# Query tiles of causal block attention moved by one 64-row block in a fused attention, gating and MLP kernel

## What is computed

```python
scores = (q @ k.T) / 8                       # per batch and head, 576 x 576
mask = (pos // 64)[:, None] >= (pos // 64)[None, :]
attn = softmax(where(mask, scores, -1e9))
x = attn @ v                                 # heads side by side: 4 x 576 x 512
h = relu(x @ w_in); u, v = h[..., :512], h[..., 512:]
v_n = (v - mean(v)) / sqrt(var(v) + 1e-6)
gated = u * (w_spatial @ v_n + b_spatial)
x = gated @ w_out
xn = (x - mean(x)) / sqrt(var(x) + 1e-6) * g_ln
out = x + relu(xn @ w_ch1) @ w_ch2
```

## Time and profile before

| what | value |
| --- | --- |
| median of three timed runs | 792.93 us (792.04 to 794.08) |
| the profiled execution | 791.29 us, of which the span of the trace is 789.5 us |
| PE busy | 778.3 us, 99% of the span |
| DVE, ACT, POOL busy | 63%, 48%, 50% |
| chain that ended last | PE 87%, DVE 6%, ACT 4%, issue 3% |

### The profile page before, as it was taken

The page is one execution under the profiler, slowest core; times in us unless marked ns, Lnnn a source line. Parts: engine busy times, 40 slices in busy tenths (PEclk is TensorE's granted clock), DMA queues, the critical chain, the costliest instruction groups (busy, mean ns, idle before and its releaser), DMA issues.

```text
span 789.5 us, 14255 instructions
## 1 busy us (share of the span) xinstructions
PE 778.3 (99%) x5088; PEld 669.1 (85%) x5088; DVE 497.2 (63%) x1028; ACT 380.5 (48%) x970; POOL 394.4 (50%) x508
## 2 busy tenths in 40 slices
PE   8999999999999999999999999999999999999998
PEld 6767888778887788879988989988898889898987
DVE  7886746366563665528767776688656687545445
ACT  5996675456564565524353333443342345333431
POOL 4886655334353243503356455656454556554541
PEclk9999999999999999999999999999999999999999
DMA  6453332312123220041263231003100000300002
GB/s 233 149 177 95 113 103 77 102 58 72 54 73 102 71 68 25 1 135 53 69 195 112 68 119 54 28 1 120 54 27 1 1 1 33 129 0 1 1 1 81
DMA packets 38149, 56.40 MB, mean 71 GB/s; under 512 B 3136, under 2 KB 20544, under 8 KB 38080
## 3 DMA queue, kind: packets, MB, share of 16 engines
q1 hardware_dynamic: 38080, 55.49, 21.5%
HBM read 46.04 MB, written 9.44 MB: 70 GB/s over the span
## 4 chain that ended last, share of the span: by engine, by line
PE 87%; DVE 6%; ACT 4%; issue 3%; POOL 0%; ACTq 0%; POOLq 0%; DVEq 0%
PE psum L1391 24%; PE psum L1392 23%; PE psum L1393 23%; PE psum L1312 5%; PE psum L1357 4%; ACT probs L808 3%; PE psum L1372 2%; DVE neg_max L1035 2%; PE psum L1377 2%; PE psum L1473 1%; DVE mix_buf L1110 1%; PE psum L1443 1%; PE psum L1426 0%; PE psum L1424 0%; DVE stats L1089 0%
## 5 line engine op out<-in xcount | busy, mean ns | idle before, releaser
L759 POOL TENSOR_TENSOR wp_r<-block,wp_r 128x256 fp32r<-128x256 f32 x168 | 133.7, 803 | 168.3 <-ACT wp_r L941 166.0
L1216 DVE TENSOR_TENSOR sums<-psum,sums 128x384 f32<-128x384 f32 x216 | 113.6, 554 | 105.8 <-PE psum L1393 105.1
L969 ACT ACTIVATE h_r<-sums 128x384 fp32r<-128x384 f32 x96 | 50.4, 526 | 228.8 <-PE psum L1393 119.1
L691 POOL TENSOR_SCALAR probs<-probs,row_inv 128x512 f32<-128x512 f32 (+4 forms) x160 | 92.5, 593 | 108.5 <-DVE row_inv L1048 108.5
L1035 DVE TENSOR_REDUCE neg_max<-psum 128x1 f32<-128x512 f32 (+4 forms) x160 | 80.7, 538 | 58.1 <-PE psum L1312 57.0
L1393 PE MATMUL psum<-w_r,h_r 128*128 128x512 f32 x288 | 114.2, 397 | 0.0
L1392 PE MATMUL psum<-w_r,h_r 128*128 128x512 f32 x288 | 113.7, 395 | 0.0
L1391 PE MATMUL psum<-operand,wp_r 128*128 128x384 f32 x336 | 113.2, 337 | 0.2 <-DVE sums L1216 0.2
L1392 PE MATMUL psum<-operand,wp_r 128*128 128x384 f32 x336 | 113.0, 336 | 0.0
L1393 PE MATMUL psum<-operand,wp_r 128*128 128x384 f32 x336 | 112.4, 334 | 0.0
L808 ACT ACTIVATE probs<-psum,neg_max 128x512 f32<-128x512 f32 (+4 forms) x160 | 89.9, 567 | 45.8 <-DVE neg_max L1035 43.6
(11 more groups left out here) (119 smaller groups left out, 1614.0 us busy)
## 6 DMA issues: line engine op xcount, KB each, us to landing
qk_raw<-qk SPq DMA_DIRECT2D x32, 576.0 KB, 4.0
block<-w_ch SPq DMA_DIRECT2D x32, 256.0 KB, 3.7
y_res<-y_scratch SPq DMA_DIRECT2D x18, 256.0 KB, 3.6
out<-y_res SPq DMA_DIRECT2D x18, 256.0 KB, 2.1
v_raw<-vN SPq DMA_DIRECT2D x16, 256.0 KB, 2.8
y_scratch<-mix_buf SPq DMA_DIRECT2D x16, 256.0 KB, 2.0
y_ring<-y_scratch SPq DMA_DIRECT2D x16, 256.0 KB, 2.7
w_raw<-w_in SPq DMA_DIRECT2D x8, 256.0 KB, 4.3
```

The costliest lines, as they stand in the source:

```text
L691: pool.tensor_scalar(probs[:, n % 2, c], probs[:, n % 2, c], row_inv[:, n % 2, AT[t]:AT[t] + 1], 1.0, ALU.mult, ALU.mult).then_inc(normed, 1)
L759: pool.tensor_tensor(wp_lo[:, n % WP], w1[i % BLOCKS][:, WEIGHT[j]], wp_hi[:, n % WP].bitcast(F32), ALU.subtract).then_inc(wp_lo_done, 1)
L1216: dve.tensor_tensor(dst, product_bank(i, j), other, ALU.add).then_inc(c_summed, 1)
```

## The change

Tiles are moved by 64 rows. Tile 0 is now the first block alone (64 queries, 64 keys, called OWN); tiles 1 to 4 have 128 rows and begin at 64, 192, 320 and 448, with 192, 320, 448 and 576 keys. `score_head` does tiles 1 to 4 in one group of ten matmuls (the keys of tile 4 beyond 512 and those of tile 2 beyond 256 are matmuls of their own, because of banks and quadrants), in banks 0 to 2, with one wait of PE for its own first results in the middle; `score_first` does tile 0's one matmul, into a mixer bank up to head 8 and the output bank later. Counters are now `scored_wide` (tiles 4, 3), `scored_narrow` (1, 2) and `scored_own`.

For t = 1 to 4 only the t full 128 x 128 pieces are transposed per tile; the 64 x 64 blocks on the diagonal of all five tiles are five small transposes, counted as tile OWN. Order of tiles: 4, 3, 1 in step 0, 2 and OWN in step 2, followed by `score_first(n + 1)`. Maxima and exponentials of head n + 1: all four big tiles before the copies in heads 0 to 7; later 4 and 3 before and 1 and 2 after them. OWN's follow in step 2. DVE copies tiles 4 and 2, ACT 3, 1 and OWN. Exponentials of tiles 1 to 4 are plain two-dimensional accesses. `attend` gets a further wait, for all exponentials of the next head. In the mixer heads GpSimd splits weights in step 0 instead of step 1. The empty slot of batches 0 and 2 moves from step 0 of the head after the eight to step 1 of the eighth head; three w groups move by one slot.

```diff
...
-KEYS = [min(P * (t + 1), S) for t in range(NT)]
+KEYS = [BLOCK + P * t for t in range(NT)]
+QUERY_AT = [0] + [BLOCK + P * (t - 1) for t in range(1, NT)]
...
-    pt = place("pt", PT_STEP * NT + P * (NT - 1))
+    pt = place("pt", S * NT)
+    pt_own = pt.rearrange("p (j n) -> p j n", j=NT)[:, :, 0:BLOCK]
...
-    DVE_TILES, ACT_TILES = [3, 1], [0, 2, 4]
+    OWN = 0
+    DVE_TILES, ACT_TILES = [4, 2], [3, 1, OWN]
     def t_place(n, t):
-        if t == NT - 1 and n < H:
-            return m_bank[:, 1, 0:NT * LAST]
-        at = KEYS[2] if t == 0 else 0
-        return t_bank[:, 0 if t in (3, 1) else 1, at:at + (t + 1) * ROWS[t]]
+        if t == 4:
+            return t_bank[:, 0, 0:4 * P]
+        if t == 3:
+            return t_bank[:, 1, 0:3 * P]
+        if t == 1:
+            return t_bank[:, 1, 3 * P:4 * P]
+        late_banks = m_bank if n < H else t_bank
+        return late_banks[0:BLOCK, 1, 0:NT * BLOCK] if t == OWN else late_banks[:, 0, 0:2 * P]
     def transposed_free(pe, n, t):
-        if t == 3 and n >= 1:
-            pe.wait_ge(t_copied_dve, len(DVE_TILES) * n)
-        elif t == 0 and n >= 1:
-            pe.wait_ge(t_copied_act, len(ACT_TILES) * n)
-        elif t == 1:
+        if t == 2 and n >= H:
-        elif t == 4 and n >= H:
+        elif t == OWN and n >= H:
-        elif t == 4 and n >= 1:
-            pe.wait_ge(t_copied_act, len(ACT_TILES) * n)
-    TILES = [3, 0, 2, 1, 4]
-    PEAKS = {3: 1, 0: 3, 2: 3, 1: 5, 4: 5}
+    TILES = [4, 3, 1, 2, 0]
-    MADE = {3: 1, 0: 3, 2: 3, 1: 4, 4: 5}
-    FIRST = 3
-    def second_in_mixer(n):
-        return n <= H
-    def second_banks(n):
-        return psum[:, 2:4, :] if second_in_mixer(n) else psum[:, 1:3, :]
+    FIRST, TURNED = 4, 3
+    WIDE = TILES[:2]
+    PEAKS = {4: 2, 3: 2, 1: 4, 2: 4, 0: 5}
+    def early(n):
+        return FIRST if n < H else len(WIDE)
+    MADE = {4: 1, 3: 3, 1: 3, 2: 4, OWN: 5}
+    SCORES = 5
     def score_of(n, t):
+        flat = psum.rearrange("p a n -> p (a n)")
-            return psum[:, 1, KEYS[2]:KEYS[2] + KEYS[0]]
-        if t == 2:
-            return psum[:, 1, 0:KEYS[2]]
-        if t == 3:
-            return psum[:, 0, 0:KEYS[3]]
-        if t == 1:
-            return second_banks(n)[:, :, pair_at(n):pair_at(n) + P]
-        return second_banks(n)[LAST:P, :, last_at(n):last_at(n) + HALF]
-    def pair_at(n):
-        return S - LAST - P if second_in_mixer(n) else 0
-    def last_at(n):
-        return 0 if second_in_mixer(n) else P
+            return (m_bank[:, 1, :] if n <= H else o_bank)[BLOCK:P, 7 * BLOCK:8 * BLOCK]
+        start = {4: 0, 3: KEYS[4], 2: KEYS[4] + KEYS[3], 1: KEYS[4] + KEYS[3] + KEYS[2]}[t]
+        return flat[:, start:start + KEYS[t]]
     def unseen():
-        for t in (3, 2, 0):
-        for n in (0, HEADS - 1):
+        return [score_of(0, t)[0:BLOCK, KEYS[t] - BLOCK:KEYS[t]] for t in TILES[:NT - 1]]
     def parts(t):
-        return slice(LAST, P) if t == NT - 1 else slice(0, P)
+        return slice(BLOCK, P) if t == 0 else slice(0, P)
+    SPARE = sum(len(r) for r in GROUP_STEPS[:H - 1])
     def groups_at(n, step):
-        return [(at // GROUPS, at % GROUPS)] if at >= 0 and in_batch(at // GROUPS, at % GROUPS) else []
+        b, g = at // GROUPS, at % GROUPS
+        if b % 2 == 0 and g >= SPARE:
+            return [(b, g - 1)] if g > SPARE else []
+        return [(b, g)] if at >= 0 else []
     def late(n, step, lag):
...
         def load_qk(n):
-                sp.wait_ge(scored_second, 4 * (n - QS + 1))
+                sp.wait_ge(scored_wide, SCORES * (n - QS + 1))
+                sp.wait_ge(scored_narrow, SCORES * (n - QS + 1))
+                sp.wait_ge(scored_own, n - QS + 1)
+                    for i in pieces_at(n - 1) if n >= H else []:
+                        split_piece(i)
                 elif step == 1 and n + 1 < HEADS:
-                    for i in pieces_at(n - 1):
+                    for i in pieces_at(n - 1) if n < H else []:
...
-                act.wait_ge(t_made, NT * (n - 2) + AT[t] + 1)
+                act.wait_ge(t_made, NT * (n - 1))
-            dst = probs[r, s, P_AT[t]:P_AT[t] + k]
-            if t in TILES[FIRST:]:
-                dst = dst.rearrange("p (a n) -> p a n", a=2)
-            act.activation(dst, score_of(n, t), ACT.Exp, bias=neg_max[r, s, AT[t]:AT[t] + 1],
+            act.activation(probs[r, s, P_AT[t]:P_AT[t] + k], score_of(n, t), ACT.Exp, bias=neg_max[r, s, AT[t]:AT[t] + 1],
         def copy_transposed(n, t):
-            w = ROWS[t]
-            src = t_place(n, t).rearrange("p (j q) -> p j q", q=w)
-            act.activation(pt_rows(t, t + 1), src, ACT.Copy).then_inc(t_copied_act, 1)
+            act.activation(pt_rows(t), t_blocks(n, t), ACT.Copy).then_inc(t_copied_act, 1)
         def output_right(n):
...
                 if step == 0:
-                        for t in TILES[:FIRST]:
+                        for t in TILES[:early(n)]:
-                    copy_transposed(n, 0)
-                    copy_transposed(n, 2)
+                    copy_transposed(n, 3)
+                    copy_transposed(n, 1)
+                    if n + 1 < HEADS:
+                        for t in TILES[early(n):FIRST]:
+                            exp_tile(n + 1, t)
                 elif step == 1:
                 elif step == 2:
-                    copy_transposed(n, 4)
+                    copy_transposed(n, OWN)
...
                 if step == 0:
-                        for t in TILES[:FIRST]:
+                        for t in TILES[:early(n)]:
-                    invert(n, 1)
+                    if n >= 1:
+                        invert(n, 1)
-                    copy_transposed(n, 3)
+                    copy_transposed(n, 4)
+                    if n + 1 < HEADS:
+                        for t in TILES[early(n):FIRST]:
+                            max_tile(n + 1, t)
                 elif step == 1:
                 elif step == 2:
+                    copy_transposed(n, 2)
-                    copy_transposed(n, 1)
...
-        def seen(n, t, half, upper):
-            query = 2 * t + upper
-            k = BLOCK * (query + 1)
-            return score(n, score_of(n, t)[HIGH if upper else LOW, 0:k], half, query, slice(0, k))
+        def seen(n, t, half, upper, start=0, end=512):
+            query = QUERY_AT[t] // BLOCK + upper
+            keys = slice(start, min(BLOCK * (query + 1), end))
+            return score(n, score_of(n, t)[HIGH if upper else LOW, keys], half, query, keys)
+        def score_head(n):
+            pe.wait_ge(q_scaled, n + 1)
+            if n >= 1:
+                pe.wait_ge(exped, NT * (n - 1) + FIRST)
+            seen(n, 2, HIGH, 1, end=256).then_inc(scored_narrow, 1)
+            seen(n, 4, LOW, 1).then_inc(scored_wide, 1)
+            seen(n, 2, HIGH, 0).then_inc(scored_narrow, 1)
+            seen(n, 4, LOW, 0).then_inc(scored_wide, 1)
+            seen(n, 3, HIGH, 0).then_inc(scored_wide, 1)
+            seen(n, 3, HIGH, 1).then_inc(scored_wide, 1)
+            pe.wait_ge(scored_narrow, SCORES * n + 2)
+            seen(n, 1, LOW, 0).then_inc(scored_narrow, 1)
+            seen(n, 2, LOW, 1, start=256).then_inc(scored_narrow, 1)
+            seen(n, 1, LOW, 1).then_inc(scored_narrow, 1)
+            seen(n, 4, HIGH, 1, start=512, end=KEYS[4]).then_inc(scored_wide, 1)
         def score_first(n):
-            pe.wait_ge(q_scaled, n + 1)
-            if 1 <= n <= H + 1:
-                pe.wait_ge(exped, NT * (n - 1) + FIRST)
-            elif n > H + 1:
-                pe.wait_ge(exped, NT * n)
-            seen(n, 3, LOW, 1).then_inc(scored_first, 1)
-            seen(n, 2, HIGH, 1)
-            seen(n, 3, LOW, 0).then_inc(scored_first, 1)
-            seen(n, 2, HIGH, 0)
-            seen(n, 0, HIGH, 1).then_inc(scored_first, 1)
-            seen(n, 0, HIGH, 0).then_inc(scored_first, 1)
-        def score_second(n):
+            pe.wait_ge(exped, NT * n)
-                pe.wait_ge(exped, NT * n + FIRST)
-            elif n >= 1:
-                pe.wait_ge(exped, NT * n)
-            for half, part in enumerate((LOW, HIGH)):
-                score(n, score_of(n, 4)[:, half, :], part, 2 * (NT - 1), slice(HALF * half, HALF * (half + 1)))
-            for half, part in enumerate((LOW, HIGH)):
-                for upper in range(2):
-                    k = BLOCK if half and not upper else P
-                    score(n, score_of(n, 1)[HIGH if upper else LOW, half, 0:k], part, 2 + upper,
-                          slice(P * half, P * half + k)).then_inc(scored_second, 1)
+                pe.wait_ge(o_right_done, n - 1)
+            score(n, score_of(n, 0), LOW, 0, slice(0, BLOCK)).then_inc(scored_own, 1)
         def transpose_tile(n, t):
-            r = ROWS[t]
-            for j in range(t + 1):
-                k = ROWS[j]
-                c = P_AT[t] + P * j
-                last = pe.transpose(place[0:k, r * j:r * (j + 1)], probs[parts(t), n % 2, c:c + k],
```

(55 more changed lines are left out.)

8 lines of the change are left out of this document (1 added, 7 removed).

## The result

The changed kernel takes 795.61 us (median of 13 runs, 793.81 to 796.27), the kernel before 792.05 us (13 runs beside it, 791.29 to 794.08): ratio 1.0036, 95% interval 1.0026 to 1.0046. It is slower by 3.6 us where 2.4 us of gain were forecast. The profiled execution took 795.69 us, its span 793.9, 4.4 above that of before.

What follows compares the result with a forecast made beforehand. PE, ACT and DVE all had little room in the early heads, PE alone bound the mixer heads; 3.7 - 4.2 - 1.6 - 0.3 = -2.4 us on 791.29 gave 788.9, as a median 790.5, range 782.5 to 796.5.

Steps and rivals of the forecast that it cites:

- Start and loop: Heads 0 to 8 up to the first mixer group: longer loop of 5.76 us per head, together +3.7 us.
- the granted clock is 1.00 in both: Premise that TensorE runs at full clock in both the early attention heads and the mixer heads; no time was added.
- The hold: In score_head PE waits for a count behind an earlier 512-column matmul: 1.76 us, 0.75 more than score_first before.
- The second case: Rival: no hold, a counter steps when its own matmul ends, score_head takes 1.45 us: 781.7 us, chance 0.15.
- Step 2: Mixer heads' step 2, with seven transposes and the 64-column score: 0.82 us instead of 1.76, a gain of 0.94.
- Waits that go: PE's waits before score groups and at the empty slot vanish, -1.6 us; that before the last batch's first group, -0.3.
- GpSimd's split at nothing: GpSimd's split of weights in step 0 instead of 1 is hidden by PE in the mixer heads and costs nothing.
- The counts' tail (3): Rival: the attention-only loop is longer as ten counts are handed out one by one, +0.38 us: 794, chance 0.20.
- ACT as the bound in step 0 (4): Rival: in mixer heads ACT's late copies delay OWN's transposes, 0.4 us in each of 15 heads: 796.5, chance 0.15.

Runs made afterwards that it cites:

- e1_warm: The changed kernel with dummy matmuls filling both idle stretches of TensorE at the start (14 instead of 6, and 8 new ones): 793.26 us, ratio 1.0014.
- e2_order: The changed kernel with the second 256-column score matmul of tile 2 issued before the first 512-column one: 785.71 us, ratio 0.9914.
- e3_warm_order: The changed kernel with dummy matmuls in both idle stretches and the second 256-column score matmul issued before the first 512-column one: 784.63 us, ratio 0.9902.
- e6_slot_back: The changed kernel with the empty slot of batches 0 and 2 back at step 0 of the head after the eight: 796.62 us, ratio 1.0054.
- e12_warm_one: The changed kernel with 14 instead of 6 dummy matmuls, filling only the first idle stretch: 793.76 us, ratio 1.0019.
- e4_before_cold: The kernel before the change without its six dummy matmuls behind the first scores, leaving TensorE idle about 2 us: 792.09 us, ratio 1.000.
- e14_warm_second: The changed kernel with dummy matmuls only in the second idle stretch, before head 2's scores: 794.51 us, ratio 1.0037.

## Why the prediction was wrong, step by step

- **Start and loop, +3.7: failed, +6.4.** The loop (5.74 for 5.76) and head 8 (6.47 us from its score group to the mixer group, for 6.5) came as worked out. The step that failed is "the granted clock is 1.00 in both": it was read from the kernel before and carried over, though my own sum put head 1's scores 1.9 us later, a time in which TensorE has nothing to do. Where 0.51 us of idle time stood, 2.26 and 1.88 came. The fall cost 2.7 us in the profiled execution (two score groups with 3.12 us from their start to what follows, where the others have 1.77) and 2.35 in the medians (e1_warm); without it the term is the 3.7 of the sum. It doesn't come alike in each run: four of the 13 runs stand at 793.8 to 794.0 us with a mean clock of 0.997 or 0.998, the other nine at 794.8 to 796.3 with 0.994 to 0.997. What decides it is open.
- **The hold, 1.76 us: right**, and e2_order shows its cause. Without it the change is a gain of 0.9%. The second case, 781.7, with the 3.1 us of the next term is 784.8; e3_warm_order, where the clock doesn't fall, took 784.6.
- **Step 2, 0.82 us: failed, 0.96.** "Another quadrant in the same mode, between 0 and 0.16 more, I take 0.06" was the mis-sized term. The seven transposes alone take 0.71, less than the 0.76 that I took from the old mix of sizes, and the score adds 0.25, outside my own bounds; the turn was excluded by a reason that no row bore out. 0.14 in 22 heads is 3.1 us. Per head score_head costs 0.76 more and step 2 gives 0.80 (1.76 less 0.96) where 0.94 was forecast: -0.04 instead of -0.19, and -0.9 instead of -4.2 in all.
- **Waits that go, -1.6 and -0.3: right**; all four are gone, and e6_slot_back shows what the moved slot covers. From the first mixer group to the end of the heads -1.7 were measured; -0.9 and -1.6 leave a remainder of +0.8.
- **GpSimd's split at nothing: failed.** Some 0.55 of this 0.8 stand in head 11 (score group to `attend` 2.02 for 1.76, from the transposes to the mixer group 1.15 for 0.85); the rest has no place of its own. I looked at whether the split would be late for its users, and not at whom GpSimd holds up while it works: `rstd` in its own queue and VectorE's subtraction. The collision was to be seen before, too, at 91.47 in VectorE's timeline of the old kernel:

```profile
91.47 1.70 DVE L1079 TENSOR_TENSOR vn_r<-mix_buf,vn_r 64x512 fp32r<-64x512 f32 x1 [2.20 <-ACT vn_r L855]
```

- **The rivals.** The counts' tail (3) is out: the loop is 5.74. ACT as the bound in step 0 (4) is out: behind head 8 no wait stands before transposes. That the time came near (4)'s, and inside the range of 782.5 to 796.5, whose upper end was (4)'s time, is luck: other causes brought it there.

The terms, +6.4, -0.9, -1.6, -0.3 and +0.8, make the 4.4 us of the spans; the last one is the remainder, so the sum is no check of it. The misses are 2.7 for the clock, 3.3 for step 2 and 0.8, which is the way from -2.4 to +4.4.

## What to carry to other kernels

Where TensorE waits on its own counter, the wait was only as early here as the longest matmul issued ahead of the last one that it counts: issue what is waited for first, and long work behind it. Where a change lengthens a loop on other engines, TensorE's idle time may have to be paid twice, for itself and for the clock behind it. And an offloaded operation is not free because it is on time: ask whom it holds up while it works.

## What the hardware showed that I had not expected

- Counts are given in the order of issue, though the matmuls of other quadrants run ahead: 0.31 us per group of ten (1.76 and 1.45), 8.6 us in all with the clock up (e3_warm_order against e1_warm), 9.9 without the dummy matmuls.
- A turn between transposes and products costs about 0.15 us there and back even with equal tile size, more than a product of 64 columns (0.11).
- Idle stretches of 1.9 to 2.3 us lowered TensorE's clock to 1.2 GHz in some executions of one program (four of 12 in e12_warm_one) and not in others; in e4_before_cold 2.05 us and in e14_warm_second 2.26 us did not in the execution that was profiled.
- VectorE's subtraction was held up for 5.7 us (6.34 for 0.69) while GpSimd went from one instruction to the next.
